# Token-ordered reads of xT in the first product, one transfer for each step's output, and edge rows of x split into 16 and 15 rows behind the bounce

## What is computed

```
w = exp(weight_gen - max); w = w / (sum(w) + 1e-9)        # (4, 4096, 8 heads, 7 taps)
x_pad = 6 zero tokens, then x                             # per sequence
attn[b, s, h, g] = sum_k w[b, s, h, k] * x_pad[b, s + k, h, g]
h = attn @ w_in                                           # (16384, 192) @ (192, 2048)
g = s * relu(h)^2 + b
out = g @ w_out                                           # (16384, 2048) @ (2048, 192)
```

## Time and profile before

| | before |
|---|---|
| median of 3 runs | 1143.09 us (1141.62 to 1144.4) |
| the profiled execution | 1143.53 us |
| its span | 1141.8 us |
| mean granted TensorE clock | 0.999 of full speed |
| PE busy | 1131.2 us, 99% of the span |
| DVE busy | 917.2 us, 80% |
| ACT busy | 721.5 us, 63% |
| POOL busy | 121.4 us, 11% |
| memory traffic | 106.76 MB, mean 94 GB/s |

### The profile page before, as it was taken

One profiled execution on the slowest core, in us unless ns is written; L12 is line 12 of the kernel. 1 busy time (PEld: TensorE's weight loads), 2 busy tenths in 40 slices (PEclk: granted clock), 3 DMA queues, 4 the chain that ended last, 5 costly groups with the idle time before them and its releaser, 6 DMA issues.

```text
span 1141.8 us, 31594 instructions
## 1 busy us (share of the span) xinstructions
PE 1131.2 (99%) x12976; PEld 1047.3 (92%) x12976; DVE 917.2 (80%) x1100; ACT 721.5 (63%) x745; POOL 121.4 (11%) x74
## 2 busy tenths in 40 slices
PE   8999999999999999999999999999999999989998
PEld 7999999999999999999999999999999999989997
DVE  8898887778787778877787877788777878777834
ACT  7777656666665566566666655665666666555663
POOL 1100011110111100111101111101111011110111
PEclk9999999999999999999999999999999999999999
DMA  8512334434334333234343343342343433333121
GB/s 254 92 53 66 93 90 107 117 73 108 80 89 117 95 86 105 75 106 117 73 108 80 89 117 90 91 106 74 105 117 74 107 80 89 89 105 102 35 59 29
DMA packets 97820, 106.76 MB, mean 94 GB/s; under 512 B 7336, under 2 KB 77876, under 8 KB 97792
## 3 DMA queue, kind: packets, MB, share of 16 engines
q1 hardware_dynamic: 94960, 103.90, 34.8%
q0 software_dynamic: 2512, 2.26, 1.3%
q10 hardware_dynamic: 320, 0.20, 0.1%
HBM read 70.62 MB, written 35.39 MB: 93 GB/s over the span
## 4 chain that ended last, share of the span: by engine, by line
PE 92%; DMA 3%; issue 2%; DVE 1%; SPq 1%; ACT 1%; POOL 0%; POOLq 0%; ACTq 0%; DVEq 0%
PE hp L1042 44%; PE op L1080 33%; PE op L1089 15%; DMA x_in<-zeros 2%; DVE scratch L641 1%; DMA xT2s<-x_bounce 0%; DMA x_bounce<-x_parts 0%; SPq L268 0%; ACT scratch L462 0%; DMA w_in<-in_weight_gen 0%; SPq L266 0%; POOL scratch L418 0%; POOL scratch L422 0%; SPq L300 0%; SPq L292 0%
## 5 line engine op out<-in xcount | busy, mean ns | idle before, releaser
L1080 PE MATMUL op<-wo,g_hi 64*128 64x384 f32 x4096 | 595.3, 356 | 0.2
L1089 PE MATMUL op<-wo,g_lo 64*128 64x192 f32 x4096 | 529.2, 247 | 0.0
L462 ACT ACTIVATE scratch<-hp 128x1024 f32<-128x1024 f32 x254 | 255.7, 1019 | 381.6 <-PE hp L1042 379.6
L759 DVE TENSOR_TENSOR g_lo<-scratch,g_hi 128x1024 fp32r<-128x1024 f32 x255 | 324.1, 1272 | 187.6 <-ACT g_hi L473 183.4
L1089 PEld LDWEIGHTS op<-wo,g_lo 64*128 64x128 f32 x4096 | 407.4, 188 | 4.4
L1080 PEld LDWEIGHTS op<-wo,g_hi 64*128 64x128 f32 x4096 | 400.2, 184 | 5.0 <-issue 0.3
L1042 PE MATMUL hp<-xT1s,w_hi 64*128 64x512 f32 x2048 | 324.6, 390 | 2.6 <-DMA xT1s<-x_bounce 2.0
L466 ACT ACTIVATE scratch<-scratch 128x1024 f32<-128x1024 f32 x255 | 269.9, 1059 | 6.0
L1042 PEld LDWEIGHTS hp<-xT1s,w_hi 64*128 64x128 f32 x2048 | 189.8, 185 | 30.6 <-DMA xT1s<-x_bounce 2.2
L1042 PE MATMUL hp<-xT1s,w_lo 64*128 64x512 f32 x1024 | 206.4, 392 | 0.0
L672 DVE TENSOR_TENSOR tap<-x_in,w_soft 128x768 f32<-128x768 f32 x186 | 177.4, 954 | 3.2
(11 more groups left out here) (83 smaller groups left out, 272.0 us busy)
## 6 DMA issues: line engine op xcount, KB each, us to landing
x_in<-in_x SPq DMA_DIRECT2D x29, 960.0 KB, 4.9
x_bounce<-x_parts SPq DMA_DIRECT2D x116, 192.0 KB, 3.7
xT1s<-x_bounce SPq DMA_DIRECT2D x29, 512.0 KB, 3.9
xT2s<-x_bounce SPq DMA_DIRECT2D x58, 256.0 KB, 4.9
out<-scratch SPq DMA_DIRECT2D x124, 96.0 KB, 1.8
w_in<-in_weight_gen SPq DMA_DIRECT2D x32, 112.0 KB, 2.1
wo_raw<-in_moe_w_out SPq DMA_DIRECT2D x4, 384.0 KB, 7.7
wo_sums<-in_moe_w_out POOLq DMA_DIRECT2D x4, 384.0 KB, 6.6
```

Of the source, the lines that this page charges most:

```text
L462: nc.scalar.activation(r[:, b, :], hp[:, PAIR * b:PAIR * (b + 1), :], ACT.Relu).then_inc(relu_done, 1)
L759: nc.vector.tensor_tensor(g_lo[:, buf, tiles, :], pair, g_hi[:, buf, tiles, :].bitcast(F32), ALU.subtract).then_inc(g_lo_ready, 1)
L1080: nc.tensor.matmul(op[:, t, 0:2 * D], g_hi[rows[h], g % 2, j, t * P:(t + 1) * P], wo[rows[h], k, :, :].rearrange("p a d -> p (a d)"), star ...
L1089: mm = nc.tensor.matmul(op[:, t, 0:D], g_lo[rows[h], g % 2, j, t * P:(t + 1) * P], wo[rows[h], k, 0, :], start=False, stop=(k == FT - 1 an ...
```

## The change

Four things change, and nothing in what is computed.

1. `first_product` reads the moving operand `xT` of the bounced steps through a view: (q t i) is read as (t q i), by token and then partition, in 16 runs of 32 columns. `by_pe` steps read as before. The output partition of the second product is then the token's own partition.
2. `out_sb` holds, for each partition, its 4 tokens in a row. `store` is one transfer of 128 partitions with 3072 bytes each, in every step; `store_by_token` goes. The last step's halves are one transfer each (1536-byte runs), the first on SP, the second on ACT's queue. The semaphore counts follow.
3. The 31 edge rows of a sequence are loaded in two transfers, of 16 and of 15 rows.
4. The wait for the edge rows and the transfer of the rest of the block (`load_rest_of_x`) stand behind the bounce that followed them.

```
-        def store_last(queue, n, t):
-            queue.dma_start(last_quarter_rows[:, n * PAIR:(n + 1) * PAIR, t * D:(t + 1) * D],
-                            out_sb[t * Q:(t + 1) * Q, n * PAIR:(n + 1) * PAIR, :]).then_inc(last_stored, FETCH)
+        def store_last(queue, n):
+            queue.dma_start(last_rows[:, n * PAIR * D:(n + 1) * PAIR * D],
+                            out_sb[:, n * PAIR:(n + 1) * PAIR, :].rearrange("p t d -> p (t d)")).then_inc(last_stored, FETCH)
...
                 for q in range(B):
                     a = q * batch_rows
-                    sp.dma_start(x_in[a + 1:a + batch_rows, block, 0:missing, :],
-                                 x_rows[a:a + batch_rows - 1, (TOK - missing) * row:TOK * row]).then_inc(x_edge_loaded[block], FETCH)
+                    for first, n in ((a + 1, batch_rows // 2), (a + 1 + batch_rows // 2, batch_rows // 2 - 1)):
+                        sp.dma_start(x_in[first:first + n, block, 0:missing, :],
+                                     x_rows[first - 1:first - 1 + n, (TOK - missing) * row:TOK * row]).then_inc(x_edge_loaded[block], FETCH)
                     sp.dma_start(x_in[a:a + 1, block, 0:missing, :].rearrange("p t d -> p (t d)"),
                                  zeros[q:q + 1, 0:missing * row]).then_inc(x_edge_loaded[block], FETCH)
-                sp.wait_ge(x_edge_loaded[block], 2 * B * FETCH)
+
+            def load_rest_of_x(block):
+                missing = PAD - STEP * block
+                sp.wait_ge(x_edge_loaded[block], 3 * B * FETCH)
                 sp.dma_start(x_in[:, block, missing:, :], x_rows[:, 0:STEP * (block + 1) * row]).then_inc(x_loaded[block], FETCH)
...
             def store(i, block=None):
                 sp.wait_ge(out_ready, i + 1)
                 block = i + AHEAD if block is None else block
-                for t in range(STEP):
-                    sp.dma_start(quarter_rows[:, :, bass.ds(block * (STEP * row) + t * row, row)],
-                                 out_sb[t * Q:(t + 1) * Q, :, :]).then_inc(out_stored, FETCH)
+                sp.dma_start(out_rows[:, bass.ds(block * (STEP * row), STEP * row)],
+                             out_sb[:, :, :].rearrange("p t d -> p (t d)")).then_inc(out_stored, FETCH)
...
             edge_loads(STEPS - 4, 0)
             bounce(STEPS - 3, 1)
+            load_rest_of_x(0)
             store(STEPS - 5)
             edge_loads(STEPS - 3, 1)
             bounce(STEPS - 2, 0)
+            load_rest_of_x(1)
             store(STEPS - 4)
             bounce(STEPS - 1, 1)
             store(STEPS - 3)
             store(STEPS - 2, 0)
-            for n in range(2):
-                sp.wait_ge(last_output_ready, n + 1)
-                for t in range(STEP // 2):
-                    store_last(sp, n, t)
+            sp.wait_ge(last_output_ready, 1)
+            store_last(sp, 0)
...
-            for n in range(2):
-                act.wait_ge(last_output_ready, n + 1)
-                for t in range(STEP // 2, STEP):
-                    store_last(act, n, t)
+            act.wait_ge(last_output_ready, 2)
+            store_last(act, 1)
...
+                def columns(part):
+                    return part if by_pe else part.rearrange("p (q t i) -> p t q i", q=P // Q, t=STEP)
...
-                        by_x1 = [(w1_hi[rows[h], f], xT1[rows[h], 0, :]), (w1_hi[rows[h], f], xT1[rows[h], 1, :]),
-                                 (w1_lo[rows[h], f], xT1[rows[h], 0, :])]
+                        by_x1 = [(w1_hi[rows[h], f], columns(xT1[rows[h], 0, :])),
+                                 (w1_hi[rows[h], f], columns(xT1[rows[h], 1, :])),
+                                 (w1_lo[rows[h], f], columns(xT1[rows[h], 0, :]))]
```

More of the change, by code:

```diff
@@ L66, in mix_and_mlp @@
     out_rows = out.rearrange("(p t) d -> p (t d)", t=TOK)
-    quarter_rows = out_rows.rearrange("(q i) c -> i q c", i=Q)
     last_block = AHEAD - 1
-    last_quarter_rows = quarter_rows[:, :, last_block * STEP * D:(last_block + 1) * STEP * D]
+    last_rows = out_rows[:, last_block * STEP * D:(last_block + 1) * STEP * D]
     w_out_tiles = moe_w_out.rearrange("(f p) d -> p f d", p=P)
@@ L280, in load_w1 @@
                                     by_parity[:, :, half, :]).then_inc(w1_loaded[g], FETCH)
-            def store_by_token(i):
-                block = i + AHEAD
-                sp.wait_ge(out_ready, i + 1)
-                for t in range(STEP):
-                    sp.dma_start(out_rows[:, (block * STEP + t) * row:(block * STEP + t + 1) * row], out_sb[:, t, :]).then_inc(out_stored, FETCH)
             def store(i, block=None):
@@ L343, in _ @@
             loads(1, 1)
-            store_by_token(0)
+            store(0)
             loads(2, 0)
             bounce(3, 1)
-            store_by_token(1)
+            store(1)
             loads(3, 1)
             bounce(4, 0)
-            store_by_token(2)
+            store(2)
             with sp.Fori(0, (STEPS - 8) // 2) as j:
@@ L366, in _ @@
             store(STEPS - 2, 0)
-            for n in range(2):
-                sp.wait_ge(last_output_ready, n + 1)
-                for t in range(STEP // 2):
-                    store_last(sp, n, t)
-            sp.wait_ge(out_stored, STEP * FETCH * (STEPS - 1))
-            sp.wait_ge(last_stored, 2 * STEP * FETCH)
+            sp.wait_ge(last_output_ready, 1)
+            store_last(sp, 0)
+            sp.wait_ge(out_stored, FETCH * (STEPS - 1))
+            sp.wait_ge(last_stored, 2 * FETCH)
         @block.gpsimd
@@ L419, in add_sums @@
                                         ALU.add).then_inc(out_added, 1)
-                pool.wait_ge(out_stored, STEP * FETCH * i)
+                pool.wait_ge(out_stored, FETCH * i)
                 pool.wait_ge(out_added, i)
@@ L796, in last_output @@
                 dve.wait_ge(out_ready, STEPS - 1)
-                dve.wait_ge(out_stored, STEP * FETCH * (STEPS - 1))
+                dve.wait_ge(out_stored, FETCH * (STEPS - 1))
                 for n in range(2):
@@ L979, in passes_of @@
                         f2 = slice((g * PAIR + j // 2) * P, (g * PAIR + j // 2 + 1) * P)
-                        by_x1 = [(w1_hi[rows[h], f], xT1[rows[h], 0, :]), (w1_hi[rows[h], f], xT1[rows[h], 1, :]),
-                                 (w1_lo[rows[h], f], xT1[rows[h], 0, :])]
-                        by_x2 = [(w2_hi[rows[h], f2], xT2[rows[h], 0, :]), (w2_hi[rows[h], f2], xT2[rows[h], 1, :]),
-                                 (w2_lo[rows[h], f2], xT2[rows[h], 0, :])]
+                        by_x1 = [(w1_hi[rows[h], f], columns(xT1[rows[h], 0, :])),
+                                 (w1_hi[rows[h], f], columns(xT1[rows[h], 1, :])),
+                                 (w1_lo[rows[h], f], columns(xT1[rows[h], 0, :]))]
+                        by_x2 = [(w2_hi[rows[h], f2], columns(xT2[rows[h], 0, :])),
+                                 (w2_hi[rows[h], f2], columns(xT2[rows[h], 1, :])),
+                                 (w2_lo[rows[h], f2], columns(xT2[rows[h], 0, :]))]
                         banks.append((j, own, by_x1, by_x2))
```

## The result

The changed kernel takes 1153.73 us (median of 6 runs, 1153.4 to 1154.05), the kernel before 1143.53 us in the runs beside it (6 runs, 1141.62 to 1145.0). The ratio is 1.0085, with an interval of 1.0075 to 1.0095: **0.85% slower**, where 0.5% faster was forecast. The profiled execution has a span of 1152.2 us, 10.4 more than before.

What follows compares the result with a forecast made beforehand. PE was taken as the bound. The profiled 1143.53 us less 5.31 for the stall and 0.1 at the end gave 1138.1; shifted to the median, 1137.7 us, 0.5% faster, range 1136.7 to 1141.2.

Steps and rivals of the forecast that it cites:

- The bound: PE's 8.72 us group rhythm sets the time; one break near step 29, from crawling edge rows, costs 5.31 us.
- Part 2, the reads: First product of bounced steps, 2088 pairs: reading xT in 16 runs of 32 columns was taken to cost 0.
- rival (b): L1042 in steps 3 to 31: reading in runs costs; one clock a jump gives 13.1 us, 1150.8; chance 0.12.
- the warm-up: PE's f32 matmuls in three 128-column runs, 0.638 us a pair: taken as showing that jumps cost nothing.
- DVE's cast: L704 on DVE, 24 runs of 32: upper bound of 1.4 ns a run, 44 us in all on PE.
- The rule on 16-byte lines: Applied to PE's reads of xT: a run of 32 f32 is eight whole lines, so the price is nothing.
- Part 1, the edge rows: Step 29's bounce: the split and the move would each remove the late start; stall and clock dip go, 5.31 us gained.
- The moved wait: DVE waiting for block 1's rest of x: a new wait of about 2.3 us, hidden by a pause, cost 0.
- rival (a): DVE's wait moves to g_lo at steps 30 and 31, POOL colliding, PE waiting: 1138.3 to 1141.2 us; chance 0.13.
- The pause of 3.34 us on DVE: DVE's idle time ahead of L759, two taps behind the new wait: claimed to hide that wait.
- Part 3, the stores: Output stores, 124 transfers of 96 KB becoming 31 of 384 KB: cost 0, nothing gained on the path.
- Part 4, the end: Last output transfer of 192 KB: landing taken as 2.3 us, 0.1 us gained, between 0.3 gained and 1.2 lost.

Runs made afterwards that it cites:

- split_only: Kernel before with only the edge rows split into 16 and 15 rows, wait and rest of x still ahead of the bounce: 1138.35 us, 0.9947.
- runs_4: Changed kernel with the split edge rows ahead of the bounce and xT read in 4 runs of 128 columns, tokens out of order: 1137.81 us.
- warm_up_f32: split_only with twelve f32 warm-up pairs instead of four, in runs of 128, 32 and 8 columns: 1141.49 us (one run).
- behind_only: Kernel before with only the wait and rest of x moved behind the bounce, edge rows still in transfers of 31 rows: 1146.53 us, 1.0023.
- edges_only: Kernel before with both edge edits, the 16 and 15 row split and the move behind the bounce, reads and stores as before: 1141.66 us, 0.9976.
- repeat_16: Changed kernel with split edge rows ahead of the bounce and the first 32 columns of xT read 16 times: 1152.75 us.

## Why the prediction was wrong, point by point

**The bound.** Right. PE's rhythm sets the time, the break costs 5.31 us, and the crawling edge rows cause it: split_only changes only these, and its span is 1136.5 us, 5.3 less than the 1141.8 of before. The price isn't the same in every execution: the four fastest of the kernel before beside the experiments took 1141.7 to 1142.0 us at a mean granted clock of 0.999 to 1.000. That is about 3.4 us above split_only, the size of the two waits alone, so in these the dip of the clock may be missing; none of them was profiled, so this isn't shown.

**Part 2, the reads: the step that failed.** It took 0 and measured 13.9 us. The mechanism of rival (b) happened, in its place, with a chance of 0.12. That its price of one clock a jump (13.1 us) came close is luck: 8 runs pay nothing and 64 pay 31 clocks. The error is in the choice between the bounds. I took the warm-up as "the row of this very engine". It differed in three ways that I hadn't weighed. Its runs are of 128 columns, a length that is free in fp32r too (runs_4). It is f32, where even runs of 8 hide (warm_up_f32). And it ran at 1.2 GHz: the reckoning of "four passes at 2.4 GHz" met 0.638 us by chance, as each row was one of a pair's two passes, at two clocks a column and half the clock; the six rows weren't six pairs. So the row couldn't have shown the price that was paid. DVE's cast, 1.4 ns a run at most, was no better a guide in size, but it was the only row with runs of 32, and 0.2 ns a jump sufficed to turn the sign. With no row of fp32r in runs, a chance near one half would have been fair.

The rule on 16-byte lines from the Trainium skill (SBUF — State Buffer, the note on cachelines) also gave nothing for runs of 32. The measurement decides: eight whole lines to a run, and 16 clocks a pair were paid.

**Part 1, the edge rows.** The stall and the dip went, as said. That each edit alone would do was half wrong: the split alone does, the move alone loses 8.2 us elsewhere (behind_only). The step that failed there: I followed the bounce's own share on the crawling engine to PE's need for xT, and didn't follow the rest of x behind it to DVE.

**The moved wait.** It is rival (a), chance 0.13, and it happened as well. The wait for block 1's rest was put at 2.3 us and measured 4.19 (edges_only 4.17). The 768 KB took 6.35 us from issue behind the loads of xT, where I had reckoned 5.7, and SP got there later (1049.67 in edges_only, reckoned 1047.8), as the wait for the block before had already made DVE late. For block 0 it was to fall to 1.4 and was 1.96 (2.08). The pause of 3.34 us on DVE, which I had named as the cover, hid the taps, but POOL's additions lost their place in it: that was named in the rival and left out of the sum. Price 3.3 us by edges_only against split_only, 2.4 in the changed kernel.

**Part 3, the stores.** Right for the changed kernel: 384 KB land in 2.4 us, nothing waits. In the old order they shorten SP's lateness by 1.5 us of issuing, which the prediction didn't see.

**Part 4, the end.** Gained 0.5 us, where 0.1 was taken and 0.3 was the best bound; the bounds came from loads of x and w (2.1 and 3.6 us), and the last stores of 192 KB landed in 1.8 and 1.9.

**Sum.** With the measured terms: 1143.53 + 13.9 - 5.3 + 2.4 - 0.5 = 1154.0, against 1154.05 for the profiled execution.

## What to carry to other kernels

A view on a matmul's moving operand is not free by default when TensorE is the bound and takes a column each clock: a price too small to see in a mean of 390 ns, paid 2088 times, beat the gain; read the distance between starts of equal groups. Before a row is taken as a bound for a new access, compare its data type, its run length and the clock at which it ran, and ask whether it could have shown a price at all. And when work is moved behind other work on a queue, follow its consumers too: here one split in 16 and 15 rows, left in its place, got the whole gain, and moving the rest of x behind the bounce as well gave 3.3 us of it back.

## What the runs showed of the hardware that I had not expected

- TensorE, moving operand of 64x512 in fp32r at 2.4 GHz: 4 runs of 128 and 8 of 64 columns are free, 16 runs of 32 cost 16 clocks a pair, 32 of 16 cost 24, 64 of 8 cost 31. Starts 128 or 256 columns apart cost the same, 16 reads of the same 32 columns one clock more (repeat_16). In f32 48 runs of 8 take no longer than 12 of 32 (0.32 us a pass of 384 columns).
- In the first microseconds PE's matmuls ran at half pace (0.64 us, then 0.32) and its weight loads too (0.34, then 0.19), though the record of the granted clock says 1.00 for this stretch: here the starts of the matmuls tell the clock, not the record.
- Transfers of 31 rows kept one engine in sixteen busy (share 0.06, 26 GB/s), and the transfer queued behind them was late: x_bounce took 10.45 us to its loads instead of 5.41 (behind_only). With 16 and 15 rows the wait for all of them ended 2 us after the last was issued (split_only).
- DVE's cast and subtraction of g took 2.3 and 2.7 us beside POOL's additions, and about 0.7 and 1.2 alone. The subtraction that had begun before POOL (1070.03 against 1070.19) took 1.22, and POOL's addition then 2.75 instead of 1.85.
